# Splitting 67-row loads, joining two batches in a request, and turning probabilities one unit later in a fused attention and feed-forward kernel

## What is computed

```python
# one attention over positions averaged in fours, repeated back to full length
q_d = q.reshape(B, H, Sd, 4, D).mean(axis=3)      # k_d, v_d alike
out_up = np.repeat(sm_attn(q_d, k_d, v_d), 4, axis=2)
# one attention in a window: |row - column| < 4
mask = np.abs(pos[:, None] - pos[None, :]) < 4
scores = np.where(mask, scale * np.matmul(q, k.transpose(0, 1, 3, 2)), -1e9)
x = out_up + softmax(scores) @ v                  # 2304 tokens x 512
xn = x / rms(x) * rms_g
x = (silu(xn @ w_gate) * (xn @ w_val)) @ w_out
return (np.maximum(x @ w_in, 0) ** 2) @ w_out2
```

## Time and profile before

| | us |
|---|---|
| median of three executions | 960.91 |
| lowest, highest | 960.46, 963.03 |
| the profiled execution, whole | 963.09 |
| the profiled execution, first to last instruction (span) | 961.3 |
| of it, until DVE's last attention work before the seam | 147 |

### The profile page before, as it was taken

How to read it: one execution, slowest core, us unless ns; L and a number is a source line. 1 busy time by engine, 2 the same in 40 slices (tenths; PEclk the granted TensorE clock), 3 DMA queues, 4 the chain that set the end, 5 groups by cost and what they waited for, 6 DMA issues and landing times.

```text
span 961.3 us, 17765 instructions
## 1 busy us (share of the span) xinstructions
PE 926.8 (96%) x6056; PEld 837.6 (87%) x6056; DVE 648.3 (67%) x960; ACT 447.9 (47%) x1149; POOL 588.7 (61%) x627
## 2 busy tenths in 40 slices
PE   5879989999999999999999999999999999999998
PEld 5657768999999999999999998989898998989896
DVE  5859995678986668876455776667875456745353
ACT  3758785644455634455444464424342324333221
POOL 2458677778778867877766775555654445453520
PEclk9979878999999999999999999999999999999999
DMA  6566211321211111111111122121112101030101
GB/s 178 180 206 210 82 35 33 89 77 54 68 45 44 45 45 45 45 45 45 44 46 54 54 69 88 44 88 45 45 36 97 45 23 44 23 110 23 45 1 65
DMA packets 57961, 63.94 MB, mean 67 GB/s; under 512 B 5904, under 2 KB 50832, under 8 KB 57488
## 3 DMA queue, kind: packets, MB, share of 16 engines
q1 hardware_dynamic: 56288, 61.63, 20.8%
q10 hardware_dynamic: 1584, 1.18, 0.4%
HBM read 58.07 MB, written 4.72 MB: 65 GB/s over the span
## 4 chain that ended last, share of the span: by engine, by line
PE 77%; DVE 3%; issue 1%; ACT 1%; POOL 0%; DMA 0%; ACTq 0%; DVEq 0%
PE bank L1437 42%; PE bank L1492 20%; PE bank L1467 14%; DVE xs L1079 1%; ACT wst L698 0%; ACT xs L739 0%; DVE vt L1146 0%; DVE prod L1152 0%; PE bank L1447 0%; DVE wst L1086 0%; POOL wst L576 0%; DMA out_dram<-xT 0%; DVE gt L1146 0%; DVE wo L1191 0%; ACT xT L822 0%
## 5 line engine op out<-in xcount | busy, mean ns | idle before, releaser
L1437 PE MATMUL bank<-xs,wst 128*128 128x384 f32 x2520 | 505.1, 340 | 4.1 <-DVE vt L1146 2.4
L1437 PEld LDWEIGHTS bank<-xs,wst 128*128 128x128 f32 x2520 | 442.7, 189 | 28.6 <-issue 8.5
L576 POOL TENSOR_TENSOR wst<-wraw,wst 128x256 fp32r<-128x256 f32 x240 | 223.9, 952 | 143.0 <-ACT wst L698 141.7
L1492 PE MATMUL bank<-wo,gs 128*128 128x512 f32 x864 | 218.4, 393 | 1.4 <-ACT xT L822 0.8
L1467 PE MATMUL bank<-hb,wo 128*128 128x512 f32 x864 | 189.1, 336 | 1.3 <-DVE hb L1164 1.3
L1492 PEld LDWEIGHTS bank<-wo,gs 128*128 128x128 f32 x864 | 160.4, 188 | 29.8 <-DVE gs L1185 1.1
L1467 PEld LDWEIGHTS bank<-hb,wo 128*128 128x128 f32 x864 | 146.0, 188 | 9.9 <-issue 1.6
L1146 DVE TENSOR_TENSOR vt<-u,bank 128x384 f32<-128x384 f32 x120 | 66.2, 552 | 126.1 <-PE bank L1437 125.8
L698 ACT CAST wst<-wraw 128x256 fp32r<-128x256 f32 x360 | 123.1, 407 | 1.9 <-DMA wraw<-w_dram 1.2
L559 POOL TENSOR_TENSOR wraw<-wraw,stage 128x256 f32<-128x256 f32 x60 | 48.9, 815 | 96.5 <-DMA wraw<-w_dram 96.5
L785 ACT ACTIVATE sig<-gt 128x384 f32<-128x384 f32 x72 | 37.9, 526 | 124.8 <-DVE gt L1146 123.7
(11 more groups left out here) (110 smaller groups left out, 1054.5 us busy)
## 6 DMA issues: line engine op xcount, KB each, us to landing
wraw<-w_dram SPq DMA_DIRECT2D x180, 128.0 KB, 2.3
stage<-w_dram SPq DMA_DIRECT2D x60, 128.0 KB, 2.1
woraw<-w_dram SPq DMA_DIRECT2D x28, 256.0 KB, 3.0
vquad<-v_dram SPq DMA_DIRECT2D x16, 288.0 KB
out_dram<-xT SPq DMA_DIRECT2D x18, 256.0 KB, 2.9
vwin<-v_dram SPq DMA_DIRECT2D x56, 70.0 KB
kp<-k_dram SPq DMA_DIRECT2D x3, 1152.0 KB, 8.6
qs<-q_dram SPq DMA_DIRECT2D x3, 1152.0 KB, 11.0
```

What stands on the lines that cost most here:

```text
L576: nc.gpsimd.tensor_tensor(b[:, 1, :], w_source(w, p), b[:, 0, :].bitcast(fp32), ALU.subtract).then_inc(wlp_done, 1)
L1437: last = mm(XY[s % 2][:, 0:HC], wst[:, u % 2, p, pw, 128 * k:128 * k + 128], xs[:, p, px, k, :], start=(p not in CONTINUES and i == 0 and ...
L1492: last = mm(ACC[t][:, :], gs[:, v % 2, m, px, 128 * t:128 * t + 128], wo[:, 2 * j + m, pw, :], start=(j == 0 and n < 18 and i == 0), stop= ...
```

## The change

1. `load_v` takes both batches of a window in one request, and the 67-row windows go as 64 rows and 3 rows.
2. `load_vquad` splits each request of 72 rows into 64 and 8.
3. `LAG_T`, `LAG_V`, `LAG_O` go from 3, 4, 5 to 4, 5, 6, and the rings of probabilities from four to five.
4. Scores use four PSUM banks up to unit 32. The fourth bank, P[7], is used for the token sums at unit 37, which therefore also wait for unit 32's exponentials.
5. `outd` moves in on-chip memory. The seam gets two calls on PE and two on ACT.

```diff
-LAG_T, LAG_V, LAG_O = 3, 4, 5
-SRING = 4
-DRING = 4
+LAG_T, LAG_V, LAG_O = 4, 5, 6
+SRING = 5
+DRING = 5
+FOUR_BANKS = 33
...
+        def v_loads(u0, u1):
+            return u1 - u0 + (u0 == 0) + (u1 == NL)
...
         def score_bank(g):
-            return SA[(g + 2) % 3]
+            return SA[g % 4] if g < FOUR_BANKS else SA[(g + 2) % 3]
+        def bank_user(g):
+            return max((f for f in range(g) if score_bank(f) is score_bank(g)), default=None)
...
-                    r0 = t0 - (QB * i - HALO)
-                    for x in range(2):
-                        src = v_d[batch0(b) + x][t0:t1, D * head0(b):D * head0(b) + GC]
-                        sp.dma_start(vwin[b % 2][r0:r0 + t1 - t0, x, i, :], src).then_inc(done, 16)
+                    r0 = QB * i - HALO
+                    for a, e in ((t0, t1),) if t1 - t0 == KW else ((t0, t0 + QB), (t0 + QB, t1)):
+                        src = v_d[batch0(b):batch0(b) + 2, a:e, D * head0(b):D * head0(b) + GC]
+                        sp.dma_start(vwin[b % 2][a - r0:e - r0, :, i, :],
+                                     src.rearrange("x r n -> r x n")).then_inc(done, 16)
...
-                        sp.dma_start(vquad[:, kt, x, :, :],
-                                     v.rearrange("(p r) n -> p r n", r=FACTOR)).then_inc(vq_in, 16)
+                        fours = v.rearrange("(p r) n -> p r n", r=FACTOR)
+                        sp.dma_start(vquad[0:64, kt, x, :, :], fours[0:64]).then_inc(vq_in, 16)
+                        sp.dma_start(vquad[64:HK, kt, x, :, :], fours[64:HK]).then_inc(vq_in, 16)
...
+            keep_output(G_ALL - 6)
+            take_turned(G_ALL - 4)
             first_copy(0)
             keep_output(G_ALL - 5)
             take_turned(G_ALL - 3)
...
                 pe.wait_ge(ss_add, 3)
+                pe.wait_ge(exp_done, FOUR_BANKS)
...
-                if g >= 3 and subtracted(g - 3):
-                    pe.wait_ge(sub_done, nth_subtracted(g - 3) + 1)
-                if g >= 3 and not subtracted(g - 3):
-                    pe.wait_ge(exp_done, g - 2)
+                old = bank_user(g)
+                if old is not None and subtracted(old):
+                    pe.wait_ge(sub_done, nth_subtracted(old) + 1)
+                if old is not None and not subtracted(old):
+                    pe.wait_ge(exp_done, old + 1)
...
+            transposes(G_ALL - 4)
+            values(G_ALL - 5)
             product(0, 0)
             transposes(G_ALL - 3)
             values(G_ALL - 4)
```

More of the change, by code:

```diff
@@ L143, in fused_kernel @@
         ssq, tmp, nrm = (sb(name, [128, CS], stack=early) for name in ("ssq", "tmp", "nrm"))
+        outd = sb("outd", [128, ND, SD], stack=early)
         early.close()
@@ L165, in fused_kernel @@
         pdT = sb("pdT", [HK, 2, 2, NQ, 2, QD], stack=att)
-        outd = sb("outd", [128, ND, SD], stack=att)
         mxl = sb("mxl", [128, SRING, NH], stack=att)
@@ L239, in fused_kernel @@
         P = [ctx.enter_context(nc.psum_tensor(f"bank{i}", [128, 512], fp32)) for i in range(8)]
-        TA, OA, SA = P[0:2], P[2:4], P[4:7]
+        TA, OA, SA = P[0:2], P[2:4], P[4:8]
         SS = P[7]
@@ L982, in sum_values @@
                 if n == 0:
-                    dve.wait_ge(vq_in, 64 * (b + 1))
+                    dve.wait_ge(vq_in, 128 * (b + 1))
                     ready(dve, pv_done, NU * b)
@@ L1384, in values @@
                     if b == 0 and i == 0:
-                        pe.wait_ge(v_part[0], 32 * V_PARTS[0])
+                        pe.wait_ge(v_part[0], 16 * v_loads(0, V_PARTS[0]))
                     if b == 0 and i == V_PARTS[0]:
-                        pe.wait_ge(v_part[1], 32 * (V_PARTS[1] - V_PARTS[0]))
+                        pe.wait_ge(v_part[1], 16 * v_loads(V_PARTS[0], V_PARTS[1]))
                     if b == 0 and i == V_PARTS[1]:
-                        pe.wait_ge(v_in[b], 32 * (NL - V_PARTS[1]))
+                        pe.wait_ge(v_in[b], 16 * v_loads(V_PARTS[1], NL))
                     if b > 0 and i == 0:
-                        pe.wait_ge(v_in[b], 32 * NL)
+                        pe.wait_ge(v_in[b], 16 * v_loads(0, NL))
                     for x in range(2):
```

## The result

| | before | changed |
|---|---|---|
| median, us | 961.45 (20 executions) | 951.37 (20 executions) |
| lowest, highest, us | 960.46, 974.56 | 949.05, 961.56 |
| profiled execution, whole; span | 963.09; 961.3 | 951.57; 949.8 |
| mean granted clock in it | 0.978 | 0.983 |

The ratio is 0.9907 (close to that of the means; the medians give 0.9895), with a 95% interval of 0.9882 to 0.9931: faster, by 10 us in the medians where 16 were forecast. The time lies 6.5 us above the forecast and 0.9 us above the upper end of its range.

The account below looks back on a forecast made before the run. Attention was taken as bound by DVE's work plus stalls for v and k, the feed-forward part by PE. 5.6 + 10.4 + 2.0 - 2.0 = 16.0 us off 963.1 gave 947.1, less 2.2 for the median: 944.9; range 938.5 to 950.5.

Parts of the forecast that it names:

- Term B: Group 1's loads: DVE's stalls of 8.86 and 1.57 us at units 18 and 19 go; gain 10.4 us (9.5 to 10.6).
- Rival 3: The split of the loads brings nothing, group 1's v is as late as before; gain 0 to 3 us, chance 0.05.
- Term A: Group 0's loads: DVE's waits of 4.16 and 1.43 us go; gain 5.6 us (4.1 to 5.8).
- at 339 GB/s they take 8.4 us: Group 0's loads: 2858 KB ahead of and with k's last part, spread over the engines, put k there at 11.5 us.
- slow bound: Group 0's loads: k there at 13 us, halfway between 339 GB/s and the 183 GB/s taken as really moved.
- What is late next?: After group 1's stall: PE some 4 us ahead, DVE still the bound, SP's requests covered by 10 us; cost nothing.
- Term C: Lags, rings and banks: half of the remaining short waits of DVE for scores go; gain 2.0 us (0 to 4).
- Term D: Seam: ACT's copies of turned units 47 and 48 come behind casts; -2.0 us at low clock, +1.0 if it holds.
- rival 1: Clock holds through the seam and the small waits go; gain 21.0 us, 939.9 us, chance 0.22.
- Rival 2: New falls of the clock or late k in attention, no gain from order; gain 11 us, 949.9 us, chance 0.17.
- Rival 4: Slower: PE idles a little per unit, the clock falls in group 2 and stays low; 977 us, chance 0.03.
- The base: Whole kernel: the median of the runs lies 2.2 us below the profiled execution, so 947.1 becomes 944.9 us.

Follow-up runs that it names:

- k_first: Changed kernel with the last part of group 0's k issued ahead of all windows; 958.05 us, ratio 0.9957.
- k_first_paced: `k_first` with SyncE waiting for unit 5's scores before issuing group 0's four-row value loads and all behind them; 951.61 us, ratio 0.9878.
- banks3: Changed kernel with three banks of scores throughout instead of four up to unit 32; 961.07 us (one execution).
- lags_only: Kernel before plus the new lags, rings and four banks, with all loads as before; 961.42 us, ratio 1.0002.
- loads_only: Kernel before plus the new loads alone, with the old lags, rings and three banks; 957.75 us, ratio 0.9924.

## Why the prediction missed

**Term B, the windows of group 1 (10.4 us): right.** The 7.61 us of the earlier trace rows are gone in every kernel with the new windows and only there are they gone; units 17 to 19 gained 9.6, since 0.4 us of short waits stand in each step now. SP's 11 requests took 10.5 us, not 5 to 9, without harm. The 28 GB/s with one engine in sixteen are gone as well. Rival 3 had a chance of 0.05 and didn't come. The Trainium skill's rule against two transfers to disjoint halves of the partitions (DMA: Bandwidth & Descriptors, Rules for kernel authors) doesn't fit this case: here the engines' share went from 0.07 to 1.01 with the new windows.

**Term A, group 0 (5.6 us): 2.2 us by its waits, 2.7 by its units. The step that failed is "at 339 GB/s they take 8.4 us", with only the 2858 KB issued up to k's last part counted.** That part was issued at 4.74 us and landed at 15.5, not 11.5. The rate itself came: 328 and 320 GB/s from 4 to 6 and from 6 to 8 us. Then it fell to 285, 264, 206 and 118 in the next stretches of 2 us, with the engines full, while SP issued the other windows from 5.17 us and `vquad` from 8.30. PE's busy time, clock, DMA share and GB/s:

```profile
9.00:13.00 4.00, 2.54 (x52) 1.00 1.12 270
13.00:17.00 4.00, 1.40 (x22) 0.94 1.15 129
```

From 2 to 15.5 us the engines moved 248 GB/s, that is 3.35 MB, where my 2858 KB (of 1024 bytes) are 2.93 MB: bytes of later loads went by before k was complete. In `k_first`, with k ahead of all windows, 328 to 345 GB/s held from 4 to 10 us and k was there at 10.2. My slow bound had the same fault: the old trace has 223 GB/s from 2 to 17.6 us, not the 183 that I called really moved, and halfway between two rates is no bound. Which of the later loads slowed k most isn't settled.

**The rest of A was there, but could not be won alone.** `k_first_paced` has no wait for k, and has units 9 and 12 at 22.3 and 29.3 us, 6.1 us ahead of the kernel before, more than the 5.6 forecast. But being early brings PE to its next block of instructions and to group 1's q earlier than the full queue delivers them. `k_first` paid 4.55 us and 21 us at the low clock; `k_first_paced` paid 2.8 us from unit 12 to unit 17 (13.8 us, 11.0 before). Under "What is late next?" I asked this of PE's scores and of SP's requests, and not of the loads for group 1's k and q, of which I wrote only "have landed at 27 us"; in the changed kernel q landed at 33.4. The program's own fetch I had not thought of.

**Term C (2.0 us, 0 to 4): right in size**, 1.8 by DVE's idle time, net of the new short waits at units 18 and 19. Where it comes from I had wrong: `banks3` leaves nothing at unit 29 to the fourth bank, and units 19 to 51 take 83.0 us before, 82.3 in `lags_only`, 82.1 in `loads_only` and 81.4 in the changed kernel, so the loads may have a part in it. Over all executions the lags and banks alone brought nothing, 961.42 against 961.53.

**Term D, the seam (-2.0 us at the low clock): right**, -2.46, by the steps named: the `pdT` copy (131.90) right behind the last cast (130.91 + 0.84), the second product at 135.06, 6.9 us behind unit 51 where it was 4.6. The low clock that I assumed was there. In eight experiments with the same order the clock was up again at the second product (rival 1's condition), and the seam took some 2.5 us less.

**Rival 2, late k and new falls of the clock (949.9, chance 0.17), is nearest to what happened**: k was late by 2.07 us with 1.29 behind it, priced at 1.5 each. Its C of 0 didn't come, and the falls were much larger than priced. I gave a new fall 1.5 us, from what stood behind the two stalls of the earlier trace rows; one from which the clock stays down for 27 to 31 us costs 9. By the heaps, seven of 20 executions paid something like that, and the range had no place for it. They also carry the median out of the range: that of the first heap alone is 950.4, within it. Rival 4 leaned on slices of nine and eight tenths from 72 to 120 us; both are nines in the earlier trace rows, which only makes its chance smaller.

**The base.** The profiled execution of before was 1.6 us above its own median of 20, that of the changed kernel 0.2. I took 2.2 off. In sum: the profiled execution lies 4.5 us above my 947.1 (A 3.4, D 0.5, C 0.2, what follows the seam 0.7, less 0.3 that the terms don't place), and the base makes the other 2.0.

## What to carry to other kernels

When a stall goes, ask for every later consumer of the same queue whether it will now be early: the next tensors, and the engine's own instruction blocks, which travel through the same DMA engines. With the DMA engines full, a gain was handed back at the next deadline in every variant here, so order the loads by deadline, and try holding some back where a fetch may be due. Count for a load also the bytes issued behind it: they share the engines. Price a gap on TensorE by what the clock does behind it, from rows at both levels, and give the range the case in which it doesn't come back: here 9 us, behind a wait of 3 to 4.

## What the runs showed of the hardware

- TensorE stopped in the middle of an accumulation group, with "issue" as its only label, for 0.55 to 4.55 us at matmul 218 or 219 in six kernels, and went on 2.5 to 2.9 us after the packet of its instruction queue had begun (16.4 to 21.3 us). In the four kernels in which PE was there at 18.4 to 18.8 us and the packet began by 16.2, it stopped for 0.05 us at most.
- Behind nearly the same wait (4.06 and 3.92 us) at nearly the same place the clock came back within 4 us in one kernel and after 30 in another, although PE was busy for all 30.00 us of it.
- Full DMA engines didn't mean high bandwidth: shares of 1.01 to 1.15 went with 129 (changed kernel, 13 to 17 us), 243 (20 to 42 us) and 339 GB/s (before, 6 to 8 us).
